# First head's q in 128 and 448 queries, its k in three pieces, second head's q_lo ahead of k_lo; next to last head's first half copied out of its bank by ScalarE alone

## The reference, cut to what matters

```python
q_pool = q.reshape(B, H, S // 2, 2, D).mean(axis=3)         # B 2, H 8, S 1152, D 64
scores = np.matmul(q_pool, k.transpose(0, 1, 3, 2)) / np.sqrt(D)
attn = np.exp(scores - np.max(scores, axis=-1, keepdims=True))
attn = attn / (np.sum(attn, axis=-1, keepdims=True) + 1e-09)
x = np.matmul(attn, v)                                       # 16 heads, 576 queries, 1152 keys each
...
```

## Time and profile before

| what | value |
|---|---|
| median of 3 runs | 1256.1 us (1255.15 to 1256.28) |
| the profiled execution | 1255.11 us |
| its span | 1253.3 us |
| TensorE busy | 1241.2 us, 99% of the span |
| VectorE, ScalarE, GpSimd busy | 748.9, 584.5, 574.2 us |

### The profile page before, as it was taken

How to read it: one execution, slowest core, us unless ns; L and a number is a source line. 1 busy time by engine, 2 the same in 40 slices (tenths; PEclk the granted TensorE clock), 3 DMA queues, 4 the chain that set the end, 5 groups by cost and what they waited for, 6 DMA issues and landing times.

```text
span 1253.3 us, 19795 instructions
## 1 busy us (share of the span) xinstructions
PE 1241.2 (99%) x7548; PEld 1139.9 (91%) x7548; DVE 748.9 (60%) x1618; ACT 584.5 (47%) x1233; POOL 574.2 (46%) x464
## 2 busy tenths in 40 slices
PE   8999999999999999999999999999999999999998
PEld 7888888999999899999999999999998998998997
DVE  6999999962223133867566466466466466466443
ACT  6999999943333234444353233233233233233221
POOL 5577777722122355745245255255255255255220
PEclk9999999999999999999999999999999999999999
DMA  7677676321110232122122122122122122122112
GB/s 171 109 120 118 123 121 122 78 61 51 33 50 26 84 96 73 40 79 85 45 77 81 40 82 81 46 79 79 49 77 77 51 77 75 54 79 71 52 35 93
DMA packets 98314, 95.29 MB, mean 76 GB/s; under 512 B 14449, under 2 KB 72305, under 8 KB 98225
## 3 DMA queue, kind: packets, MB, share of 16 engines
q1 hardware_dynamic: 97904, 93.51, 29.8%
q10 hardware_dynamic: 320, 0.59, 0.2%
HBM read 88.59 MB, written 2.40 MB: 73 GB/s over the span
## 4 chain that ended last, share of the span: by engine, by line
PE 93%; ACT 5%; DVE 1%; issue 1%; DMA 0%; POOL 0%; SPq 0%; DVEq 0%; POOLq 0%
PE bank L1028 12%; PE bank L1030 11%; PE bank L1029 11%; PE bank L1183 10%; PE bank L1182 10%; PE bank L1184 10%; PE bank L907 5%; PE bank L1005 4%; PE bank L1006 4%; PE bank L1007 4%; PE bank L882 4%; PE bank L920 3%; PE bank L921 3%; ACT probs L1276 2%; ACT pT_hi L1199 2%
## 5 line engine op out<-in xcount | busy, mean ns | idle before, releaser
L1669 DVE TENSOR_TENSOR c<-bank,c 128x256 f32<-128x256 f32 (+1 forms) x448 | 197.3, 456 | 280.3 <-PE bank L1030 268.1
L840 POOL TENSOR_TENSOR w_lo<-w_raw,w_hi 128x512 fp32r<-128x512 f32 x128 | 163.7, 1299 | 288.0 <-ACT w_hi L1199 288.0
L1183 PE MATMUL bank<-w_lo,h_hi 128*128 128x512 f32 x576 | 225.1, 391 | 0.0
L1182 PE MATMUL bank<-w_hi,h_hi 128*128 128x512 f32 x576 | 225.1, 391 | 0.0
L1184 PE MATMUL bank<-w_hi,h_lo 128*128 128x512 f32 x576 | 224.4, 390 | 0.0
L1394 ACT ACTIVATE h_hi<-c 128x256 fp32r<-128x256 f32 (+1 forms) x256 | 112.5, 445 | 160.1 <-DVE c L1669 159.8
L1184 PEld LDWEIGHTS bank<-w_hi,h_lo 128*128 128x128 f32 x576 | 108.2, 188 | 22.9
L1182 PEld LDWEIGHTS bank<-w_hi,h_hi 128*128 128x128 f32 x576 | 108.3, 188 | 20.8
L1183 PEld LDWEIGHTS bank<-w_lo,h_hi 128*128 128x128 f32 x576 | 108.3, 188 | 20.1
L1544 DVE TENSOR_REDUCE part_min<-bank 128x1 f32<-128x256 f32 (+2 forms) x216 | 114.6, 558 | 20.0 <-PE bank L921 13.3
L1199 ACT ACTIVATE c<-bank 128x256 f32<-128x256 f32 (+1 forms) x64 | 26.2, 410 | 214.6 <-PE bank L1030 214.6
(11 more groups left out here) (150 smaller groups left out, 2993.7 us busy)
## 6 DMA issues: line engine op xcount, KB each, us to landing
w_raw<-in_moe_w SPq DMA_DIRECT2D x64, 512.0 KB, 3.6
w_raw<-in_moe_w SPq DMA_DIRECT2D x64, 256.0 KB, 3.1
q_raw<-in_q SPq DMA_DIRECT2D x30, 288.0 KB, 6.2
k_raw<-in_k SPq DMA_DIRECT2D x30, 288.0 KB, 7.6
wo_raw<-in_moe_w_out SPq DMA_DIRECT2D x16, 384.0 KB, 3.5
v_raw<-in_v SPq DMA_DIRECT2D x16, 288.0 KB, 5.8
gv_raw<-in_moe_w_gate SPq DMA_DIRECT2D x12, 256.0 KB, 2.9
gv_raw<-in_moe_w_val SPq DMA_DIRECT2D x12, 256.0 KB, 3.2
```

The source lines that it names most:

```text
L840: ins = nc.gpsimd.tensor_tensor(w2_lo[:, u % 2, c], w2_raw[:, c], f32(w2_hi[:, u % 2, c]), ALU.subtract)
L1182: nc.tensor.matmul(bank[:, 3 + i], hh, wh, start=first, stop=False)
L1183: nc.tensor.matmul(bank[:, 3 + i], hh, wl, start=False, stop=False)
L1669: nc.vector.tensor_tensor(dst[:, 0:w], bank[:, (u + b) % 3, 0:w], other[:, 0:w], ALU.add).then_inc(done, 1)
```

## The change

- The first head's q comes in 128 and 448 queries. Its k comes in three pieces of 256, 384 and 512 keys (FIRST_KPIECES), each with a wait of its own on ScalarE, and TensorE waits for one piece ahead of each block of tile 0. ScalarE issues six transfers in place of four.
- q_hi of the other 448 queries moves ahead of tile 0 in ScalarE's queue; their q_lo moves from tile 1 to tile 0 on VectorE, and TensorE wants it for tile 1. GpSimd waits until all three k_lo are done before it sums those 448 queries.
- GpSimd does head 1's q_lo ahead of its k_lo. In the other pairs the order stays.
- 30 transposes of constants in place of 36 ahead of tile 0.
- The last pair takes its steps from AV_STEPS like the others (6, 6, 6 in tiles 4 to 6). Head 14's first half leaves its bank in ScalarE's tile 6 by two copies, own rows and other rows; VectorE's add_rows then reads SBUF alone and moves to tile 8, and the value product of the second half waits for ScalarE (tail_shifted).

```diff
-AV_STEPS_LAST = (9, 9, 9, 9, 9, 9, 0, 9, 9)
-WARM_UP, WARM_TILE = 36, 9
-Q_BEGIN = 2 * PARTS
+WARM_UP, WARM_TILE = 30, 9
+Q_BEGIN = PARTS
 KPIECES = ((0, 640), (640, 1152))
+FIRST_KPIECES = ((0, 256), (256, 640), (640, 1152))
...
         def k_there(h, pieces):
-            return k_lo_done[h > 0], 2 * (h - 1) + pieces if h else pieces
+            return k_lo_done[h > 0], 2 * (h - 1) + pieces if h else 1 + pieces
...
                 if p >= 1:
                     denominators(h - 1)
-                split_k(h + 1)
-                pool.wait_ge(*k_there(h + 1, 2))
-                q_lo_part(h + 1)
+                    split_k(h + 1)
+                    pool.wait_ge(*k_there(h + 1, 2))
+                    q_lo_part(h + 1)
+                else:
+                    pool.wait_ge(q_summed[1], 1)
+                    q_lo_part(1)
+                    split_k(1)
                 split_v(h, 0)
...
             pool.wait_ge(q_loaded[0], 32)
+            pool.wait_ge(*k_there(0, 2))
             nc.gpsimd.tensor_tensor(q_sum[0][:, rest], q_raw[0][:, 0, rest], q_raw[0][:, 1, rest],
                                     ALU.add).then_inc(q_summed[0], 1)
...
                     if h == NHEAD - 1 and u == 1:
                         pe.wait_ge(o_copied, 2 * h)
+                    elif h == LAST and u == 1:
+                        pe.wait_ge(tail_shifted, 1)
...
                     if g == 0:
                         pe.wait_ge(q_begin_lo_done, 1)
+                        pe.wait_ge(k_lo_done[0], 1)
                     else:
                         pe.wait_ge(*q_there(h))
-                    pe.wait_ge(*k_there(h, 1))
+                        pe.wait_ge(*k_there(h, 1))
...
                 score(pair, i, 0)
+                if g == 0:
+                    pe.wait_ge(*k_there(0, 1))
                 score(pair, i, 1)
...
                 if h >= LAST:
+                    if h == LAST and u == 0:
+                        copy(o_all[h % ORING][rows_of(a), cols], bank[rows_of(a), 7, 0:QHALF])
                     copy(tail_other(a)[:, cols], bank[rows_of(1 - a), o_bank(h, u), 0:QHALF]).then_inc(tail_shifted, 1)
...
-                if i == 0 and pair == 0:
-                    q_hi_part(0)
                 if i == 0:
                     q_hi_part(h + 1)
...
-                if i == (6 if h < LAST else 5):
+                if i == 6:
                     o_out(h, 0, 0)
...
-            for piece, done in enumerate((k_begin_loaded, k_loaded[0])):
-                k0, k1 = KPIECES[piece]
+            for piece, done in enumerate((*k_begin_loaded, k_loaded[0])):
+                k0, k1 = FIRST_KPIECES[piece]
...
-            k_hi_part(0, 0)
-            k_hi_part(0, 1)
+            for piece in range(3):
+                k_hi_part(0, piece)
+            q_hi_part(0)
             all_tiles(tile)
...
+                own = o_all[h % ORING][rows_of(a), cols]
+                part = own if h == LAST and u == 0 else bank[rows_of(a), o_bank(h, u), 0:QHALF]
+                nc.vector.tensor_tensor(own, part, tail_other(a)[:, cols], ALU.add).then_inc(o_copied, 1)
...
-                if g == 1:
+                if g == 0:
                     dve.wait_ge(q_hi_done, 1)
                     first_q_lo(slice(Q_BEGIN, QLEN), q_lo_done[0])
-                if h == NHEAD - 1 and i == 6:
+                if h == NHEAD - 1 and i == 8:
                     add_rows(LAST, 0, 0)
...
-            split_first_k(0)
-            split_first_k(1)
+            for piece in range(3):
+                split_first_k(piece)
```

More of the change, by code:

```diff
@@ L242, in build @@
         q_loaded = [sem(f"q_loaded{a}") for a in range(2)]
-        k_begin_loaded = sem("k_begin_loaded")
+        k_begin_loaded = [sem(f"k_begin_loaded{n}") for n in range(2)]
+        k_first_hi_done = sem("k_first_hi_done")
         q_begin_loaded = sem("q_begin_loaded")
@@ L397, in k_of @@
         def k_of(h, piece):
-            k0, k1 = KPIECES[piece]
+            k0, k1 = (KPIECES if h else FIRST_KPIECES)[piece]
             return k_st[h % KRING][:, k0:k1], k_raw[h % 2][:, k0:k1]
@@ L720, in split_k @@
                     st, raw = k_of(h, piece)
-                    pool.wait_ge(k_hi_done, 2 * h + piece + 1)
+                    pool.wait_ge(k_hi_done, 2 * h - 2 + piece + 1)
                     nc.gpsimd.tensor_tensor(st[rows_of(0)], raw[rows_of(0)], f32(st[rows_of(0)]),
@@ L949, in tile @@
                         fill_p(g - 1, j)
-                steps = AV_STEPS_LAST if pair == NHEAD // 2 - 1 else AV_STEPS
                 if i < COMMON and pair >= 1:
-                    for n in range(sum(steps[:i]), sum(steps[:i + 1])):
+                    for n in range(sum(AV_STEPS[:i]), sum(AV_STEPS[:i + 1])):
                         av(2 * pair - 1, n)
@@ L956, in tile @@
                 if i >= COMMON:
-                    for n in range(sum(steps[COMMON:i]), sum(steps[COMMON:i + 1])):
+                    for n in range(sum(AV_STEPS[COMMON:i]), sum(AV_STEPS[COMMON:i + 1])):
                         av(2 * pair, n)
@@ L1213, in k_hi_part @@
             def k_hi_part(h, piece):
-                if h == 0 and piece == 0:
-                    act.wait_ge(k_begin_loaded, 32)
+                if h == 0 and piece < 2:
+                    act.wait_ge(k_begin_loaded[piece], 32)
                 else:
                     act.wait_ge(k_loaded[h % 2], 32 * (h // 2) + 32)
-                nc.scalar.activation(*k_of(h, piece), ACT.Copy, scale=split_scale[:, 0:1]).then_inc(k_hi_done, 1)
+                nc.scalar.activation(*k_of(h, piece), ACT.Copy,
+                                     scale=split_scale[:, 0:1]).then_inc(k_hi_done if h else k_first_hi_done, 1)
             def p_hi(g, j):
@@ L1493, in split_first_k @@
                 st, raw = k_of(0, piece)
-                dve.wait_ge(k_hi_done, piece + 1)
+                dve.wait_ge(k_first_hi_done, piece + 1)
                 lo_part(st[rows_of(0)], raw[rows_of(0)], st[rows_of(0)], k_lo_done[0])
```

2 lines of the change are left out of this document (removed).

## The result

| | median | profiled execution | its span |
|---|---|---|---|
| before | 1255.86 us (1254.93 to 1256.83, 12 runs) | 1255.11 us | 1253.3 us |
| after | 1258.76 us (1255.41 to 1260.23, 12 runs) | 1259.49 us | 1257.7 us |

The ratio is 1.0022, with a 95% interval of 1.0013 to 1.0031: **the change costs 2.9 us**, where a gain of 1.6 was forecast. In the profiled pair the difference is 4.4 us.

A forecast was written before the change was run, and what follows sets the result against it. TensorE bounds the kernel (93% of the span), so time is won only where it waits. Gains of 1.30 and 0.30 less 0.05 make 1.55 us, giving 1254.5 us against the median, range 1252.8 to 1256.1.

The forecast's parts named there:

- the landing of the third piece: Start, head 0: k's last transfer, issued at 3.88, lands at 7.9 us, within bounds of 6.9 to 9.1.
- q_hi at 5.8: Start, ScalarE: head 0's q_hi starts at 5.8 us, after six issues and the table load, 1.3 sooner than 7.13.
- First exp at 11.3, k_lo at 9.4: Start, tile 0: third k_lo ends at 9.4 against 10.48, first exp at 11.3 against 12.22; 0.9 us by itself.
- The new collision: Start: VectorE's q_lo(0) waits out GpSimd's 576-column sum; tile 1 starts at 12.85 against 13.15, gaining 0.30 us, not 0.9.
- q_lo ahead of k_lo, 1.30: Tile 4: GpSimd's q_lo of head 1 no longer holds it, so it starts on its exp; 1.30 us gained.
- Last pair, 0.05 lost: Last pair: steps fill TensorE's idle before tile 7, copy and addition move; between 0.1 gained and 0.2 lost, taken as 0.05 lost.
- Warm-ups, v_split: Start: 30 warm-up transposes end near 7.4 us and cost nothing; v_split stays covered by 0.3 to 0.4 us.
- Rival (2), late k: Start: third piece of k lands at 9.1, tile 1 starts 0.3 us late; 1255.15, or 1255.6 with v_split late; chance 0.11.
- Rival (3), the clock: TensorE's clock falls while idle 1.35 us before tile 1; 2.7 to 5 lost less 1.6 gained, 1257.2 to 1259.5; chance 0.05.

The follow-up runs named there:

- e7: Kernel after, with the last pair's first-half addition moved out of tile 8 to just ahead of the second half's; 1258.17 us, ratio 1.0022.
- e12: Kernel after, with the first head's k in two pieces as before, q still in 128 and 448 queries; 1254.93 us, ratio 0.9998.
- e15: Two-piece k variant of the kernel after, with ScalarE issuing k's second piece only behind the eighth warm-up transpose; 1258.8 us, ratio 1.0030.
- e9: Kernel before, with head 1's q_lo ahead of its k_lo, GpSimd starting it only after VectorE's q_lo of head 0; 1253.96 us, ratio 0.9989.
- e3: Kernel before, with only head 1's q_lo moved ahead of its k_lo on GpSimd; 1255.6 us, ratio 0.9995.
- e6: Kernel after, with 30 more transposes of constants between tile 0's second and third score blocks; 1258.11 us, ratio 1.0022.
- e1: Kernel after, with the old last pair; 1258.58 us, ratio 1.0021.
- e14: Kernel after with two-piece k, the old last pair, and GpSimd's sum of the second head's q behind VectorE's q_lo; 1253.21 us, ratio 0.9982.
- e2: Kernel before, with only the new last pair; 1256.74 us, ratio 1.0008.
- e11: Kernel after, second head's q issued after the first 128 queries are summed, old last pair, GpSimd's sum behind VectorE's q_lo; 1256.08 us, ratio 0.9999.
- e10: Kernel after, with SyncE issuing the second head's q only once VectorE has summed the first 128 queries; 1257.48 us, ratio 1.0009.

## Why the prediction was wrong

The step that failed is the landing of the third piece: "head 0's q and k are 1.18 MB both before and after, so the last of them should land about when it did, 2.63 + 5.2 = 7.85. I take 7.9." Same bytes, but not the same company. Before, ScalarE's last transfer of k was issued at 2.6, a microsecond ahead of the second head's q, which SyncE issues at 3.57 in both kernels. With six issues the last one comes at 3.9, behind it, and the engines carry both. The kernel after's profile has no record of that landing, only the k_hi that it released at 11.05, 7.1 us behind the issue at 3.92. e7 has the same start, and its record is whole. Tile k_raw, ScalarE's transfers in e7:

```profile
DMA to landing us min/median/max: 2.2/3.5/7.0
```

7.0 us from issue to landing lies outside the 3.0 to 5.2 that the forecast had taken as bounds from the earlier trace rows. Those bounds came from transfers that all ran ahead of the second head's q, so they were no bounds for one behind it. The same part of the forecast says that the DMA engines have "nothing to spare"; it was used for the bytes of head 0 and not for whose bytes they carry at 4 us. k_hi started 11.05 − 7.9 = 3.15 us late against it.

Point by point:

- *q_hi at 5.8*: right (5.87), and so were the six issues and the table load behind them. It bought nothing, as k decides. The halved transfer of q has no gain of its own either: with the two pieces of k issued at once beside it (e12) it was there at 6.53, against 6.67; it came by 4.55 in the kernel after and by 5.47 in e15, where k's second piece is issued late.
- *First exp at 11.3, k_lo at 9.4*: wrong in the kernel after (14.72). The steps behind the landing were right: e12, where the piece lands in time, has 11.36 and 9.43.
- *The new collision*: right in kind, q_lo 0.94 us instead of 0.62. Its size was low where k lands in time: in e12 q_lo is 1.00 us longer than alone (1.62 against 0.62) and tile 1 starts at 13.16 where 12.85 was forecast, so nothing of the gain was left in place of 0.30.
- *q_lo ahead of k_lo, 1.30*: right as a mechanism; e9 shows 1.29. The forecast said that the moved q_lo "lies in time that GpSimd has idle" and priced nothing for it; in the kernel before's own timing it meets VectorE's q_lo(0) there, and e3 shows 0.6 us lost to that. In the kernel after VectorE's q_lo had gone to tile 0, out of its way, and tile 4 gave back 1.2.
- *Last pair, 0.05 lost*: right to within 0.1 without the meeting, 1.4 with it in the profiled pair. The failed words are "VectorE's addition (0.44) moves from tile 6 to tile 8 ... the rest, up to 0.2". The addition's operand moved from the bank into SBUF, and so it now shuts out and is shut out by GpSimd, a rule that the forecast itself cited for the start.
- *Warm-ups, v_split*: free, as forecast; neither releases TensorE anywhere. The warm-ups ended at 6.66, not near 7.4, since their faster spacing began at 4.7 us and not at 6.4.
- *Rival (2), late k*: the mechanism that happened, with a size too small by 2 us (9.1 against 11.05), for the reason above. *Rival (3), the clock*: it happened as well, from an idle time of 3.68 us, which is indeed longer than any in the rows; it lay inside tile 0 and not behind it; the fall was priced at 2.7 to 5 us and measured 1.1 (e6 against the kernel after), and nothing in e1 and e7. The rates that the forecast read for the two levels, 5.5 and 14 records per us, count every record that touches a window; by their starts the transposes stand 0.21 and 0.11 us apart. Its 1257.2 to 1259.5 holds the median, but by luck: most of the loss was rival (2)'s and the last pair's.

The sum for the profiled pair: late piece, with the collision behind it, 2.49 (e6's tile 2), clock 1.14 (3.63 − 2.49), tile 3 0.10, q_lo ahead −1.20, drift from tile 4 to 71 0.44, last pair 1.43: 4.40 us. The median's loss is smaller, 2.9. How it divides no trace shows, and the executions differ: of the kernel after's twelve, the one whose mean clock was 1.000 took 1255.41, and the other eleven, at 0.997 to 0.999, 1257.0 to 1260.2. There is no trace of that one, and the clock alone doesn't explain it, since e6 took 1257.5 to 1259.6 with the clock at 1.000 throughout. That most of it is the late third piece rests on medians as well: 1.0022 with it, 0.9998 without (e12), 1.0030 with the late issue alone (e15).

## What to carry to other kernels

A transfer's landing depends on what other queues have issued by then: when one is split, ask whether its last piece is now issued behind somebody else's bulk load, and take bounds only from transfers with the same neighbours. When an operand moves from a bank into SBUF or an operation moves on VectorE or GpSimd, look at what the other one is doing in that very microsecond, for two such operations take turns and the later one bears the whole wait; a semaphore that orders them (e9, e14) is worth more than the reordering alone. And a start that is fed late can be paid twice, since TensorE's clock may fall in the gap: 1.1 us here in one profile, nothing in two others.

## What the runs showed of the hardware

- A VectorE operation with two SBUF operands, begun while GpSimd works in SBUF, ends 0.3 to 0.5 us after GpSimd's: 0.44 became 0.74 to 2.22, 0.49 became 1.28, 0.62 became 0.94 to 1.66. Begun 0.03 us ahead of GpSimd's, it kept its time, and GpSimd's took 2.67 instead of 2.40 (e2). One that reads a bank kept its time.
- Idle time alone did not decide whether the clock fell. It fell behind 1.92 us in e11 and 2.21 in e10, and not in e12, which idled 2.31 ahead of tile 0 and 1.92 ahead of tile 1. Nor was the low level equally long where it fell: until past 18 us in the kernel after, until 16 us in e1 and e7, which have the same start. What else counts is open.
- The stretch in mid-kernel isn't quite steady. In single executions ScalarE and VectorE, then TensorE, stand still together for 0.2 to 1.5 us. Ten of the seventeen profiles have such stalls (seven have none, the kernel before's among them), and always at tile 31, 40, 49, 58, or 66 or 67, nine tiles apart, so at the same place of a pair. e11 at tile 67:

```profile
239.75 1.49 DVE L1557 TENSOR_REDUCE part_min<-bank 128x1 f32<-128x256 f32 x3 [1.61 <-PE bank L931]
239.88 0.77 ACT L1212 ACTIVATE pT_hi<-bank 128x256 fp32r<-128x256 f32 x2 [1.05 <-PE bank L892]
```

  Both are put down to TensorE, whose first scores had been in their bank since 238.2. The cause is open, and these stalls are why one profile's end says less than its tile 4.
